# Attention and two gated MLP layers on one core: both up-projections by seven block products instead of eight

## What is computed

```python
# attention: q, k, v (4, 8, 576, 64), f (4, 8, 576)
scores = q @ k.T / 8 + cum(log f)[query] - cum(log f)[key]      # causal
attn = softmax(scores) @ v                                      # -> x (2304, 512)
# layer 1
xn = x / sqrt(mean(x * x) + 1e-6) * rms_g
x = (silu(xn @ w_gate) * (xn @ w_val)) @ w_out                  # 512 -> 1536 -> 512
# layer 2
x = silu(x @ w_in) @ w_out2                                     # 512 -> 2048 -> 512
```

## Time and profile before

| | |
|---|---|
| median of 3 runs | 1060.02 us (1058.48 to 1061.4) |
| the profiled execution | 1060.7 us |
| its span, first to last instruction | 1058.9 us |
| PE, PEld busy | 98%, 89% of the span |
| DVE, ACT, POOL busy | 34%, 34%, 23% |
| granted clock of PE | 1.0 of full speed (2.4 GHz) throughout |

### The profile page before, as it was taken

The page is one execution under the profiler, slowest core; times in us unless marked ns, Lnnn a source line. Parts: engine busy times, 40 slices in busy tenths (PEclk is TensorE's granted clock), DMA queues, the critical chain, the costliest instruction groups (busy, mean ns, idle before and its releaser), DMA issues.

```text
span 1058.9 us, 17512 instructions
## 1 busy us (share of the span) xinstructions
PE 1038.1 (98%) x6190; PEld 946.7 (89%) x6190; DVE 358.4 (34%) x836; ACT 358.0 (34%) x819; POOL 247.7 (23%) x258
## 2 busy tenths in 40 slices
PE   5999999999999999999999999999999999999998
PEld 4777766899999999999999998999999999999997
DVE  5777768435232232241241242111121121111111
ACT  4777777432131241141141122322322222232222
POOL 3777754476001010020001677000000000000000
PEclk9999999999999999999999999999999999999999
DMA  7676565032000000000000333000000000000000
GB/s 222 198 211 210 167 191 146 1 100 60 1 0 0 0 0 0 0 0 0 0 0 3 92 105 100 1 1 30 0 30 0 0 30 0 30 0 0 30 1 30
DMA packets 29051, 52.63 MB, mean 50 GB/s; under 512 B 5648, under 2 KB 9744, under 8 KB 29008
## 3 DMA queue, kind: packets, MB, share of 16 engines
q1 hardware_dynamic: 29008, 52.07, 16.4%
HBM read 47.26 MB, written 4.79 MB: 49 GB/s over the span
## 4 chain that ended last, share of the span: by engine, by line
PE 94%; DVE 2%; ACT 1%; issue 1%; DMA 1%; SPq 0%; DVEq 0%; ACTq 0%
PE banks L979 20%; PE banks L981 20%; PE banks L980 20%; PE banks L1065 6%; PE banks L1066 6%; PE banks L1064 6%; PE banks L926 4%; PE banks L894 4%; PE banks L865 4%; PE banks L868 1%; PE banks L904 1%; PE banks L875 1%; DMA qk_raw<-qk_t 0%; DVE x_sb L700 0%; PE banks L877 0%
## 5 line engine op out<-in xcount | busy, mean ns | idle before, releaser
L979 PE MATMUL banks<-xn,w_main 128*128 (+1 forms) x576 | 193.6, 336 | 1.7 <-POOL w_kept L409 1.6
L981 PE MATMUL banks<-xn,w_main 128*128 (+1 forms) x576 | 193.2, 335 | 0.0
L980 PE MATMUL banks<-xn,w_main 128*128 (+1 forms) x576 | 192.9, 335 | 0.0
L790 DVE TENSOR_TENSOR gated_sb<-banks,act_sb 128x384 f32<-128x384 f32 x72 | 40.1, 557 | 227.2 <-PE banks L981 203.3
L979 PEld LDWEIGHTS banks<-xn,w_main 128*128 128x128 f32 x576 | 108.2, 188 | 5.2 <-issue 2.0
L981 PE MATMUL banks<-xn,w_kept 128*128 (+1 forms) x336 | 112.7, 335 | 0.0
L979 PE MATMUL banks<-xn,w_kept 128*128 (+1 forms) x336 | 112.6, 335 | 0.0
L980 PE MATMUL banks<-xn,w_kept 128*128 (+1 forms) x336 | 112.5, 335 | 0.0
L980 PEld LDWEIGHTS banks<-xn,w_main 128*128 128x128 f32 x576 | 108.1, 188 | 2.5
L981 PEld LDWEIGHTS banks<-xn,w_main 128*128 128x128 f32 x576 | 108.1, 188 | 0.0
L565 ACT ACTIVATE hid<-gated_sb 128x384 fp32r<-128x384 f32 x72 | 37.9, 526 | 156.2 <-DVE gated_sb L790 156.2
(11 more groups left out here) (149 smaller groups left out, 2019.3 us busy)
## 6 DMA issues: line engine op xcount, KB each, us to landing
w_stage<-w SPq DMA_DIRECT2D x68, 256.0 KB, 2.7
qk_raw<-qk_t SPq DMA_DIRECT2D x16, 576.0 KB, 3.4
cum_b<-cum_dram SPq DMA_DIRECT2D x32, 288.0 KB, 6.1
v_sb<-v_p SPq DMA_DIRECT2D x16, 320.0 KB, 4.7
cum_t<-cum_dram SPq DMA_DIRECT2D x32, 144.0 KB, 5.5
out<-out_sb SPq DMA_DIRECT2D x18, 256.0 KB, 2.0
qk_raw<-qk_t SPq DMA_DIRECT2D x32, 16.0 KB, 3.5
f_sb<-f SPq DMA_DIRECT2D x1, 72.0 KB, 2.1
```

The source lines that it names most:

```text
L979: nc.tensor.matmul(dst, w_hi_part, m_hi, start=start, stop=False)
L980: nc.tensor.matmul(dst, w_hi_part, m_lo, start=False, stop=False)
L981: return nc.tensor.matmul(dst, w_lo_part, m_hi, start=False, stop=stop)
```

## The change

**Spans and halves.** The work of both layers goes by 3 spans of 768 tokens (two tiles). Each span is worked in two halves of the hidden blocks: `NHALF` is 12 halves, g = 0 to 5 in layer 1 and 6 to 11 in layer 2. A half is a few up cycles (3 in layer 1, 2 in layer 2) and then its down-projection, 6 chunks of 8 x 3 matmuls of 384 columns in layer 1, 8 chunks of 6 x 3 matmuls of 512 in layer 2. All is written out, without loops. The second half's down sums are added to the first's in `x_sb`.

**Seven products.** A cycle handles two units u (in layer 1 gate and value of two hidden blocks, in layer 2 four hidden blocks). For a unit the weights are a 2x2 of blocks A (two hidden blocks of 128 x two halves of the 512 inputs), the span's x is a 2x2 of blocks B (two input halves x two tiles), and the four outputs are made of seven products of 6 matmuls (2 chunks x 3 passes) instead of eight. For that S1 to S4 are sums of weight blocks, T1 to T4 sums of x blocks:

```diff
+STAGED = {"A21": 0, "A11": 1, "A12": 2, "A22": 3, "S3": 0, "S2": 1, "S4": 2, "S1": 3}
+M_ORDER = ("M1", "M6", "M2", "M7", "M5", "M4", "M3")
+CYC1 = NSPAN * NF1 // 2
+NCYC = CYC1 + NSPAN * NF2 // 4
+PREP_IN_CYCLE = {n: n + 1 for n in range(NCYC - 1) if n == 0 or n not in [CYCLES_OF[g][0] for g in range(NHALF)]}
+PREP_IN_DOWN = {g: CYCLES_OF[g][-1] + 2 for g in range(NHALF - 1)}
 # POOL
+            for g in range(NHALF):
+                norm_next = g < HALVES1 and g % 2 == 0 and span_of(g) + 1 < NSPAN
+                for k, n in enumerate(CYCLES_OF[g]):
+                    m = PREP_IN_CYCLE.get(n)
+                    if m is not None:
+                        w_raw(m, 0)
+                        w_raw(m, 1)
+                        w_sums(m, 0)
+                    hid_lo(n, 0)
+                    if m is not None:
+                        w_sums(m, 1)
+                    hid_lo(n, 1)
+                    hid_lo(n, 2)
+                    if n == CYCLES_OF[g][-1]:
+                        w_down(PIECE_OF[g])
+                    hid_lo(n, 3)
+                    if n == CYCLES_OF[g][-1]:
+                        w_down(PIECE_OF[g] + 1)
+                    if norm_next and k < 2:
+                        for c in range(DC):
+                            if (k == 1 and c >= 2) if n < 2 else k == 0:
+                                square_sums(span_of(g) + 1, c, slice(0, SPAN))
+                            elif n == 0 and c < 2:
+                                square_sums(span_of(g) + 1, c, slice(0, SPAN))
+                m = PREP_IN_DOWN.get(g)
...
+                elif m is not None:
+                    x = (g + 1) // 2
+                    xb_lo(x, "B11")
+                    xb_lo(x, "B21")
+                    w_down(PIECE_OF[g] + 2)
+                    xb_lo(x, "B22")
+                    w_down(PIECE_OF[g] + 3)
+                    w_raw(m, 0)
+                    w_down(PIECE_OF[g] + 4)
...
 # ACT
+            def m1_copy(n, u):
+                act.wait_ge(multiplied, made(n, "M1", u))
+                wait(act, c21_made, 2 * (n - 1) + u + 1)
+                nc.scalar.activation(first_sum(u), product(n, "M1", u), ACT.Copy).then_inc(m1_out, 1)
+                for n in CYCLES_OF[g]:
+                    units = range(1 if first_layer(n) else 2)
+                    m1_copy(n, 0)
+                    if m is not None:
+                        w_raw(m, 0)
+                    m1_copy(n, 1)
+                    if m is not None:
+                        w_raw(m, 1)
+                    for u in units:
+                        silu(n, 0, u)
+                    if m is not None:
+                        w_sums(m, 0)
+                    for u in units:
+                        hid_high(n, 0, u)
+                    if m is not None:
+                        w_sums(m, 1)
...
 # DVE
+            def s_sums(n, u):
+
+                dve.wait_ge(wu_split, 4 * n + 1 + u)
+                at = 8 * n + 4 * u
+                nc.vector.tensor_tensor(staged(u, "S1"), staged(u, "A21"), staged(u, "A22"), ALU.add).then_inc(s_made, 1)
+                dve.wait_ge(s_made, at + 1)
+                nc.vector.tensor_tensor(staged(u, "S3"), staged(u, "A11"), staged(u, "A21"), ALU.subtract).then_inc(s_made, 1)
...
+            def make_c11(n, u):
+                dve.wait_ge(multiplied, made(n, "M2", u))
+                output_free(n, 0, u)
+                nc.vector.tensor_tensor(output(u, 0), first_sum(u), product(n, "M2", u), ALU.add).then_inc(c11_made, 1)
...
+            def finish(n, i):
+
+                if first_layer(n):
+                    dve.wait_ge((c11_made, c22_made, c21_made, c12_made)[i], 2 * n + 2)
+                    dve.wait_ge(silu_done, nth(n, i))
+                    nc.vector.tensor_tensor(output(1, i), output(1, i), output(0, i), ALU.mult).then_inc(gated, 1)
+                else:
+                    dve.wait_ge(hid_hi, nth(n, i, 0))
+                    nc.vector.tensor_tensor(hid_of(n, 0, i, 1), output(0, i), f32(hid_of(n, 0, i, 0)),
+                                            ALU.subtract).then_inc(lo_by_dve, 1)
...
+                    add_m6(n, 0)
+                    add_m6(n, 1)
+                    if m is not None:
+                        s_sums(m, 0)
+                    make_c11(n, 0)
+                    make_c11(n, 1)
+                    if norm_next and k == 2:
+                        take_mean(span_of(g) + 1)
+                    add_m7(n, 0)
+                    finish(n, 0)
+                    if m is not None:
+                        s_sums(m, 1)
+                    add_m7(n, 1)
+                    make_c22(n, 0)
+                    add_m5(n, 0)
+                    make_c22(n, 1)
+                    add_m5(n, 1)
+                    finish(n, 1)
+                    make_c21(n, 0)
+                    make_c21(n, 1)
+                    finish(n, 2)
+                    make_c12(n, 0)
+                    make_c12(n, 1)
+                    finish(n, 3)
...
 # PE
+            def down(g, c):
+
+                d = PIECE_OF[g] + c
+                pe.wait_ge(wd_split, d + 1)
...
+                for b in range(BANKS_OF[g]):
+                    if first:
+                        product_read(*TURNS[g][len(TURNS[g]) - 8 + b])
```

More of the change, by code:

```diff
@@ new lines @@
+X_AT = {"B11": 0, "B21": 1, "B22": 2, "T2": 3, "T3": 4, "T1": 5, "T4": 6}
+B_ORDER, T_ORDER = ("B11", "B21", "B22"), ("T2", "T3", "T1", "T4")
+T_STEPS = {"T1": 1, "T3": 2, "T2": 3, "T4": 4}
+M_ORDER = ("M1", "M6", "M2", "M7", "M5", "M4", "M3")
+OUTPUTS = ("C11", "C22", "C21", "C12")
+CYC1 = NSPAN * NF1 // 2
+NCYC = CYC1 + NSPAN * NF2 // 4
+HALVES1 = 2 * NSPAN
+NHALF = 2 * HALVES1
+CYCLES_OF = [range(3 * g, 3 * g + 3) if g < HALVES1 else range(CYC1 + 2 * (g - HALVES1), CYC1 + 2 * (g - HALVES1) + 2)
+             for g in range(NHALF)]
@@ new lines, with first_layer, span_of, made @@
+PREP_IN_DOWN = {g: CYCLES_OF[g][-1] + 2 for g in range(NHALF - 1)}
+SQUARES_PAIR, SUMS_PAIR, MEAN_PAIR = 5, 10, 11
+PREP_PAIR = 1
+def first_layer(n):
+    return n < CYC1
+def span_of(g):
+    return g // 2 % NSPAN
+def made(n, m, u):
+    return 14 * n + 2 * M_ORDER.index(m) + u + 1
+TURNS = []
+for _g in range(NHALF):
+    TURNS.append([])
+    for _n in CYCLES_OF[_g]:
+        for _m in M_ORDER:
+            if _m == "M7" and _g < HALVES1 - 2 and _g % 2 == 0 and _n == CYCLES_OF[_g][-1]:
+                TURNS[_g] += [(_n, "mean", 0), (_n, "mean", 1)]
+            TURNS[_g] += [(_n, _m, 0), (_n, _m, 1)]
@@ L417, in square_sums, with w_raw @@
[L417 to L428, removed]
+            def w_raw(n, u):
+                pool.wait_ge(wu_hi, 4 * n + 1 + u)
+                nc.gpsimd.tensor_tensor(wu[n % 2][:, u, 1, 0:RAW], stage_u[:, u, BLOCK:], f32(wu[n % 2][:, u, 0, 0:RAW]),
+                                        ALU.subtract).then_inc(wu_split, 1)
@@ new lines, in _, with square_sums @@
+            steps = 0
+            def square_sums(span, c, cols):
+                nonlocal steps
+                x = x_sb[:, c, span * SPAN + cols.start:span * SPAN + cols.stop]
+                total, square = (norm_tmp(span, i)[:, cols] for i in range(2))
+                wait(pool, sq_step, steps)
+                nc.gpsimd.tensor_tensor(square if c else total, x, x, ALU.mult).then_inc(sq_step, 1)
+                steps += 1
+                if c:
+                    pool.wait_ge(sq_step, steps)
+                    nc.gpsimd.tensor_tensor(total, total, square, ALU.add).then_inc(sq_step, 1)
+                    steps += 1
@@ L723, in _ @@
                     x_out(p - 2, 1)
+                if p == NPAIRS:
+                    t_lo(0, "T2")
                 if p > 0:
@@ new lines, in take_mean, with add_m6 @@
+            def take_mean(span):
+                dve.wait_ge(mean_done, span + 2)
+                for t in range(2):
+                    nc.vector.tensor_scalar(norm_tmp(span, 0)[:, t * TT:(t + 1) * TT], product(CYCLES_OF[2 * span - 2][-1], "mean", t),
+                                            RMS_EPS, None, ALU.add).then_inc(mean_out, 1)
+            def add_m6(n, u):
+                dve.wait_ge(multiplied, made(n, "M6", u))
+                dve.wait_ge(m1_out, 2 * n + u + 1)
+                wait(dve, c12_made, 2 * (n - 1) + u + 1)
+                nc.vector.tensor_tensor(second_sum(u), first_sum(u), product(n, "M6", u), ALU.add).then_inc(m1_m6, 1)
```

995 lines of the change are left out of this document (620 added, 375 removed).

## The result

The changed kernel takes 1260.2 us (4 runs, 1258.3 to 1261.2) against 1060.7 for the one before: 1.188 times as long, 95% interval 1.185 to 1.191. Slower, as forecast, but 60 us more than the 1200 of the forecast and 25 us beyond the range's upper end.

The account below looks back on a forecast made before the run. PE bounded the kernel before; after, DVE and POOL on a shared port would set its pace in preparing cycles. 998.4 + 6 (attention) + 148 (layer 1) + 55 (layer 2) = 1207, forecast 1200 us, range 1062 to 1235.

Parts of the forecast that it names:

- PE's instructions: Up products in both layers: 2880 matmuls become 2520, 360 x 0.173 = 62.3 us less, leaving 998.4 us.
- The port and the walk: Preparing cycles: DVE, held by POOL's port use and queue order, takes 21.3 us against PE's 14.55; +148 layer 1, +55 layer 2.
- cycles of "about 20": Sign in the profile after: each half's first cycle 14.6 us on PE, the others about 20.
- two prices of ACT: ACT operations priced from a slope: about 0.85 us for 768 columns and 1.06 for 1024.
- the matmuls still take 0.173 and 0.233: Sign for PE: matmuls of 384 and 512 columns keep 0.173 and 0.233 us after the change.
- the weights of cycle 0 are put at nothing: Attention pairs 1 to 4: DVE and ACT have 30% free, so preparation costs nothing; without that cover 7 us.
- the guess and the end of attention: Attention: longer first guess and Newton operations some 2 us more, DVE operations after the last pair 4 at most; together +6.
- the sum of 1207: Whole kernel: 998.4 + 6 + 148 + 55 = 1207 us, 1206 to the median.
- The discount from 1207 to 1200: Whole kernel: forecast lowered to 1200 us because a walk with every small wait rounded up may be somewhat dense.
- The chains without the port: Rival: POOL hardly blocks DVE, a preparing cycle has 15.4 us, only W0 is late; 1067 us, chance 0.12.
- the saving is kept: Rival: DVE and POOL work falls into each other's waits, PE stays the bound; 1004 us, chance 0.10.
- a second walk: Forecast for regrouped S sums: a preparing cycle about 18 us, 3.3 less in each of 18; near 1200 us.

Follow-up runs that it names:

- order_once2: Changed kernel with S sums grouped, first down weights and squares earlier, attention reordered, and up weights prepared only in each layer's first span: 1068.8 us.
- port_alone: Separate kernel timing DVE and POOL operations alone and together: 32 DVE additions 10.8 us, 8 POOL subtractions 18.4, both together 28.0.
- narrow_s: Changed kernel with DVE's S sums cut to 32 of 256 columns, order and waits unchanged: 1213.6 us.
- order: Changed kernel with both units' S sums together behind the second add_m7, w_sums rounded after all eight, POOL's hidden block 0 before them: 1218.9 us.
- fill_long2: Changed kernel with 97 idle matmuls on PE before a half's first down chunk (45 in the first half, none in the last): 1251.4 us.
- att2: Changed kernel with only attention reordered: cycle 0's S sums ahead of qk_round on DVE, w_sums one pair later: 1249.7 us.
- fill: Changed kernel with idle PE matmuls before the first down chunk (60 in layer 1, 30 in its first half, 55 in layer 2, none last): 1262.0 us.

## Why the prediction was right and wrong

- **PE's instructions.** Right: 62 us fewer; in `order_once2` the up parts come out at 84 x 0.173 us a cycle.
- **The port and the walk.** Right in kind and size: 21.3 forecast, 21.5 measured for a cycle; up parts of all halves 617 us forecast, 627.5 measured (tables' sums). The port is shown by `port_alone` and by an operation of 0.19 us that takes 2.23 in `narrow_s`; that the order makes it costly, by `order`, where the same work saves 41 us. One of the signs was off: cycles of "about 20" on PE for all but the first of a half. The second has 14.6 too, but for g = 0 and 2, and DVE's lag reaches PE mostly as the wait for the first down piece. And two prices of ACT don't follow from their rows: 0.53 us for 384 columns and 0.60 for 512 give 0.75 for 768 and 0.89 for 1024, not 0.85 and 1.06. The measured means are 0.84 and 1.05, so the walk had the right sizes by a working that doesn't give them.
- **Where it failed, first: the price of a matmul behind a wait.** The prediction had "the matmuls still take 0.173 and 0.233". Behind the rests of 11 to 12 us in front of the first chunks PE works at 1.2 GHz for 3 to 6 us, at 0.32 us for a matmul of 384 columns. The down parts were forecast at 374 us and took 405. From the spacing of their matmuls the lower clock costs about 33 us there (in g = 0 and 2 also behind the waits for W4 and W5 inside the phase). Against it, an undisturbed down part of layer 2 has 32.7 us (g = 8 of `order_once2`) and not 33.5, a matmul of 512 columns 0.227 and not 0.233: 5 us less. `fill_long2` takes most or all of the rest in front of the first chunk away in every half but the last. By the same reading the cost in the down parts falls from 33 to 18 us, of which 8.8 reach the time; the rest of this sum is read from the trace and not tried.
- **Second: "the weights of cycle 0 are put at nothing"** in attention. 30% idle time of an engine was taken as cover; but the queue is in order. S2 was held behind POOL's 2.92 us operation, and ACT's `w_sums` had to wait for it. `att2` gives back 10.5 us by order alone (11.9 at the first product). The prediction named 7 for lost cover.
- **Third: the guess and the end of attention**, +2 and +4 forecast. With the weights' part gone (`att2`) the first product still comes 6.8 us later than before the change, about 6 of it in the pairs with mean, guess and Newton, and no run takes these apart. The changeover (first product to the first M2) has 2.5 more, where 4 were forecast. All attention: 11.9 + 6.8 + 2.5 = 21.2 instead of 6.
- Together: 31 us for the down parts, 15 for attention and 10 for the up parts (these 10 are not explained) make 56, to 2 us the 54 by which the sum of 1207 was short. The discount from 1207 to 1200 went the wrong way, and the range's upper side stood for errors of the walk alone, not for a cost that the sum left out.
- **Rivals.** "The chains without the port" and "the saving is kept" did not happen. Even with up weights for nothing in two spans, the saving isn't reached.

What stays open: in layer 1 `order` gained half of what a second walk said, and I didn't work out why.

## What to carry to other kernels

Fewer matmuls pay only while the engines that feed them stay out of sight: count the added work as time on a shared resource (here DVE's work with both operands in SBUF plus POOL's, 645 of 787 us) and not as busy shares of single engines, and walk once through the queues in the order written. Such a walk came within 1% for a cycle from rows of a kernel that had none of it. Where it shows PE resting for several microseconds, price the matmuls behind the rest at the lower clock as well, and where an operation goes into a queue with idle time, ask what runs on the shared port at that moment.

## What the runs showed of the hardware

- The granted clock fell within the rests of PE in front of the first chunks, and came back only when PE had worked again for a while. In the changed kernel it stood at 0.50 at the end of each rest of 11 to 12 us in front of a first chunk (0.50 from 396 to 398 us, with no matmul), and stayed there for 3 to 6 us of work. In `fill`, where idle matmuls left rests of 4.2 to 5.8 us in these ten places, it was down in every one of them before the chunk began; `fill` gained nothing, and `fill_long2`, with 0.5 us left in most, did.
- A DVE copy from SBUF to SBUF is held by POOL's subtractions like an addition: 23.7 us for 32 instead of 6.6. POOL's memset doesn't hold DVE's additions (10.9 us for 32, as alone), and ACT's copies don't either (10.9). The Trainium skill (SBUF — State Buffer, section "SBUF: two separate sides") has the first, in that a DVE operation in a mode with two ports, as a plain fp32 copy in SBUF has it, takes the shared pair of ports; and the second, in that two SBUF inputs meet only a POOL operation that reads SBUF. The rows agree with both.
